# Weaving the units of two expert layers within a step, and a down projection by points

## The reference

```python
h = mab(I, x);  x1 = mab(x, h)                       # attention, x: (2, 11456, 128)
logits = xn @ en.T / tau                             # first router
out[mask] = gate_w[mask, None] * (relu(x[mask] @ w1[e]) @ w2[e])   # F = 1024
logits = x @ w_gate + modality_bias[modality_id]     # second router, same expert form
```

## Time and profile before

| | |
|---|---|
| median of 3 runs | 1131.33 us (1130.93 to 1133.27) |
| the profiled execution | 1135.07 us |
| its span, first to last instruction | 1133.3 us |
| TensorE, VectorE, ScalarE, GpSimd busy | 88%, 67%, 61%, 18% of the span |
| a step of the loop | 19.25 us, 42 of them in the loop |

### The profile page before, as it was taken

How to read it: one execution, slowest core, us unless ns; L and a number is a source line. 1 busy time by engine, 2 the same in 40 slices (tenths; PEclk the granted TensorE clock), 3 DMA queues, 4 the chain that set the end, 5 groups by cost and what they waited for, 6 DMA issues and landing times.

```text
span 1133.3 us, 28294 instructions
## 1 busy us (share of the span) xinstructions
PE 1001.1 (88%) x6551; PEld 510.2 (45%) x6551; DVE 758.2 (67%) x2211; ACT 686.4 (61%) x1656; POOL 198.7 (18%) x438
## 2 busy tenths in 40 slices
PE   5266446589999999999999999999999999999886
PEld 4144312245445454555455554454554545554342
DVE  3144457566767777777777686767677777777563
ACT  3134346356666676666666666666666766666453
POOL 2691000211111111111111111111111111111000
PEclk9688769699999999999999999999999999999998
DMA  4976665000110101010000010001001010100000
GB/s 129 275 225 218 215 215 172 22 20 28 27 28 19 36 19 32 23 29 26 27 27 27 27 27 27 27 27 27 27 19 35 18 33 22 29 25 20 21 11 20
DMA packets 68615, 64.70 MB, mean 57 GB/s; under 512 B 9570, under 2 KB 60770, under 8 KB 68568
## 3 DMA queue, kind: packets, MB, share of 16 engines
q1 hardware_dynamic: 68568, 64.11, 19.0%
HBM read 40.55 MB, written 23.55 MB: 57 GB/s over the span
## 4 chain that ended last, share of the span: by engine, by line
PE 81%; SPq 6%; DMA 5%; issue 3%; DVE 2%; ACT 2%; POOL 1%; ACTq 0%; DVEq 0%; POOLq 0%
PE y L1224 42%; PE up L1247 22%; PE up L1237 7%; DMA stage<-in_moe_w 2%; SPq L301 2%; DMA GW<-in_x 2%; PE y L1311 2%; SPq L303 2%; PE up L1163 1%; PE TB L1271 1%; PE SM L1295 1%; SPq L316 1%; PE SM L1283 1%; SPq L310 1%; PE TB L1259 1%
## 5 line engine op out<-in xcount | busy, mean ns | idle before, releaser
L811 DVE SCALAR_TENSOR_TENSOR hlo<-up,hhi 128x500 f16<-128x500 f32 x736 | 490.2, 672 | 205.5 <-ACT hhi L560 203.0
L560 ACT ACTIVATE hhi<-up 128x500 f16<-128x500 f32 x736 | 415.5, 586 | 143.3 <-PE up L1237 75.9
L1247 PE MATMUL up<-ytb,W1B 128*128 (+1 forms) x1104 | 277.7, 382 | 17.4 <-issue 14.8
L1224 PE MATMUL y<-hhi,W2A 128*128 128x500 f16 x736 | 217.1, 376 | 1.1 <-DVE hlo L811 1.1
L1224 PE MATMUL y<-hhi,GW 128*128 128x500 f16 x736 | 216.0, 374 | 0.5 <-DVE hlo L811 0.4
L1247 PEld LDWEIGHTS up<-ytb,W1B 128*128 x1104 | 108.6, 99 | 155.8 <-issue 48.2
L1237 PE MATMUL up<-E4T,GW 128*128 (+1 forms) x368 | 138.4, 380 | 0.0
L1224 PE MATMUL y<-hlo,W2A 128*128 128x500 f16 x368 | 137.8, 374 | 0.0
L1224 PE MATMUL y<-hlo,GW 128*128 128x500 f16 x368 | 137.6, 374 | 0.0
L476 POOL TENSOR_TENSOR st<-ss,root 125x4 f32<-125x4 f32 x46 | 46.8, 1018 | 374.5 <-ACT TB L592 374.5
L1224 PEld LDWEIGHTS y<-hhi,W2A 128*128 x736 | 67.8, 97 | 66.6 <-issue 15.5
(11 more groups left out here) (158 smaller groups left out, 1053.5 us busy)
## 6 DMA issues: line engine op xcount, KB each, us to landing
x_turned<-GW SPq DMA_DIRECT2D x46, 250.0 KB, 4.1
xth<-x_turned SPq DMA_DIRECT2D x46, 250.0 KB, 2.6
out<-yout SPq DMA_DIRECT2D x46, 250.0 KB
GW<-in_x SPq DMA_DIRECT2D x46, 240.0 KB
stage<-in_moe_w SPq DMA_DIRECT2D x16, 512.0 KB, 4.2
W1B<-in_moe_w SPq DMA_DIRECT2D x8, 512.0 KB, 7.2
w2s<-in_moe_w SPq DMA_DIRECT2D x8, 512.0 KB, 3.9
GW<-in_x SPq DMA_DIRECT2D x46, 10.0 KB
```

The costliest lines, as they stand in the source:

```text
L560: nc.scalar.activation(hhi[:, (u % UP) * CT:(u % UP + 1) * CT], ups[u % UP][:, 0:CT], ACT.Relu).then_inc(s["hi_done"], 1)
L811: nc.vector.scalar_tensor_tensor(hlo[:, o:o + CT], ups[u % UP][:, 0:CT], 0.0, hhi[:, o:o + CT], ALU.max, ALU.subtract).then_inc(s["lo_done ...
L1224: ins = mm(y[:, 0:CT], W[:, bass.ds(woff + (fb * 2 * C + o), C)], h[:, k * CT:(k + 1) * CT], start=opens and fb == 0 and n == 0, stop=fb = ...
L1247: ins = mm(ups[k][:, 0:CT], W1B[:, bass.ds(woff + (wl * F + fb * P), P)], ytb[:, bass.ds(yoff + yl * CW, CT)], start=n == 0, stop=n == 2)
```

## The change

1. The order of TensorE's units in a step with both layers becomes 0, 1, 8, 2, 3, 9, 4, 5, 10, 6, 7, 11, 12, 13, 14, 15: layer one's first three units stand between layer two's. Buffers and tasks go by position, no longer by unit.
2. Layer two's down takes the hidden activations as the stationary operand and the weights as the moving one: 12 matmuls of 128 columns with a weight load each, in place of 3 of 500. Its output has points on partitions, so `yT`, its copy and the four transposes go.
3. ScalarE's squares are split over positions 4 and 5; the result's four parts stand at 13 (two), 14 and 15; exps moves from 13 to 11. The factor 1/S_OUT moves into `coef` on VectorE.
4. The second router moves to position 1. `hhi` and `hlo` get 4 columns of padding a slot, cleared once by GpSimd ahead of the pipeline.

```diff
+        hhi, hlo = (sb(n, [P, UP * CW], f16)[:, :] for n in ("hhi", "hlo"))
-        yT = sb("yT", [P, CT])[:, :]
+        WOVEN = (0, 1, 8, 2, 3, 9, 4, 5, 10, 6, 7, 11, 12, 13, 14, 15)
...
-            for m in (ytb, E4T):
+            for m in (ytb, E4T, hhi, hlo):
                 nc.gpsimd.memset(m[:, :], 0.0).then_inc(s["pads_cleared"], 1)
... (ScalarE)
-                def squares():
+                def squares(h):
                     act.wait_ge(s["att_done"], p + 1)
-                    for j in range(TJ):
+                    for j in range(h * TJ // 2, (h + 1) * TJ // 2):
...
-                def yt(after):
-                    act.wait_ge(s["pass_done"], after)
-                    nc.scalar.activation(yT[:, :], y2[:, 0:CT], ACT.Copy, scale=1.0 / S_OUT).then_inc(
...
+                def result(j, after):
+                    if j == 0:
+                        act.wait_ge(s["gate_steps"], CG * (c + 3))
+                        act.wait_ge(s["out_free"], c + 1)
+                        act.wait_ge(s["pass_done"], after)
+                    ins = nc.scalar.activation(yout[:, j * C:(j + 1) * C], y2[0:TQ, j * C:(j + 1) * C], ACT.Copy,
+                                               scale=coef[:, bass.ds(parity(c) * TJ + j, 1)])
...
-                            8: [lexps] if rx or ry else [], 10: [lambda: yt(after())] if l2 else [],
-                            13: [exps] if xq else [], 15: [result] if l2 else []}
+                            5: [lambda: squares(1)] if rx else [], 8: [lexps] if rx or ry else [],
+                            11: [exps] if xq else [], 13: part(0) + part(1), 14: part(2), 15: part(3)}
... (TensorE)
+                def down_by_point(woff, opens):
+                    def down(fb, k):
+                        if fb == 0 and opens:
+                            pe.wait_ge(s["result_ready"], c + 1)
+                        for n, (h, o) in enumerate(((hhi, C), (hhi, 0), (hlo, 0))):
+                            for j in range(TJ):
+                                ins = mm(y2[:, j * C:(j + 1) * C], h[:, k * CW + j * TQ:k * CW + j * TQ + P],
+                                         W2B[:, bass.ds(woff + (fb * 2 * C + o), C)],
...
-                def out_transposes():
...
-                tasks = {1: when(rx, first_router), 2: when(ry, second_router),
-                         7: when(xq, scores), 8: when(joint, counts), 12: when(l2, out_transposes)}
+                tasks = {1: when(rx, first_router) + when(ry, second_router),
+                         7: when(xq, scores), 8: when(joint, counts)}
...
+                        if n == 2:
+                            us = [us[k] for k in WOVEN]
```

More of the change, by code:

```diff
@@ L608, in exps, with part @@
                         s["chunk_exp"], 1)
[L610 to L617, removed]
-                def tasks(after):
-                    return {1: [e4t] if rx else [], 4: [squares] if rx else [],
-                            8: [lexps] if rx or ry else [], 10: [lambda: yt(after())] if l2 else [],
-                            13: [exps] if xq else [], 15: [result] if l2 else []}
+                def result(j, after):
[5 more added lines that the diff above has]
+                                               scale=coef[:, bass.ds(parity(c) * TJ + j, 1)])
+                    if j == TJ - 1:
+                        ins.then_inc(s["result_ready"], 1)
+                def tasks(after):
+                    def part(j):
+                        return [lambda: result(j, after())] if l2 else []
+                    return {1: [e4t] if rx else [], 4: [lambda: squares(0)] if rx else [],
+                            5: [lambda: squares(1)] if rx else [], 8: [lexps] if rx or ry else [],
+                            11: [exps] if xq else [], 13: part(0) + part(1), 14: part(2), 15: part(3)}
                 def step(mixed):
@@ L956, in factors @@
                         hold(v, "result_ready", c + 1)
-                        tell(nc.vector.tensor_tensor(coef[:, now], gs[:, 1, 1, :], c1[:, now], ALU.mult), "gate_steps")
+                        tell(nc.vector.scalar_tensor_tensor(coef[:, now], gs[:, 1, 1, :], 1.0 / S_OUT, c1[:, now], ALU.mult,
+                                                            ALU.mult), "gate_steps")
                     else:
@@ L1179, in units @@
             def units(base, us, tasks, start=()):
-                for u, up, _down, _last in us[:UP]:
-                    up(u % NF, u % UP).then_inc(s["up_done"], 1)
+                first = us[0][0]
+                for k, (u, up, _down, _last) in enumerate(us[:UP]):
+                    up(u % NF, k).then_inc(s["up_done"], 1)
                 for task in start:
@@ L1192, in units @@
                         w, up = us[k + UP][:2]
-                        up(w % NF, w % UP).then_inc(s["up_done"], 1)
-                    for task in tasks.get(u, ()):
+                        up(w % NF, k % UP).then_inc(s["up_done"], 1)
+                    for task in tasks.get(first + k, ()):
                         task()
@@ L1249, in up @@
                         return ins
-                    def before():
-                        pe.wait_ge(s["result_ready"], c + 1)
-                    return up, down_of(W2B, woff, y2, opens, before if opens else None)
+                    return up, down_by_point(woff, opens)
                 def e4():
```

33 lines of the change are left out of this document (15 added, 18 removed).

## The result

| kernel | median us | runs | ratio to before (95% interval) |
|---|---|---|---|
| before | 1131.32 | 1130.93 to 1133.27 | |
| changed | 1191.05 | 1189.42 to 1194.47 | 1.052 (1.049 to 1.0551) |

A forecast was written before the change was run, and what follows sets the result against it. TensorE was taken as the bound, with a new wait for the last `hlo` at each step's end: 44 steps x 0.60 = 26.4, less 1.7 at the edges, +24.7, so 1131.3 becomes 1156 us, range 1118 to 1182.

The forecast's parts named there:

- The routers at position 1 find `e4t` done: Middle of the step: `e4t` is ready at t = 3.35, the routers need it at 4.55; no cost entered.
- A down by points 0.68: Layer two's downs on TensorE: 0.68 us each, +0.05 apiece, +0.40 a step (from +0.1 to +2.9).
- The rival with 0.0825 a pair: Weight loads don't hide in long runs: 0.99 a down, 2.5 a step more, 1265 us; chance 0.09.
- Idle time ahead of position 14: End of the step: result parts delay relu 14 and 15, so TensorE idles 0.84 us for the last `hlo`.
- The rival in which the parts don't hold relu up: End of the step: ScalarE does the result's parts under TensorE's work; +0.15 a step, 1136 us; chance 0.12.
- The next step's start: Step's end: next first up 1.69 us after the last `hlo`, at 19.86, so each step is 0.60 longer.
- The stalls at 7 and 8 gone: Middle of the step: the weave removes TensorE's two waits for `hlo`, 0.26 us.
- Transposes gone, -0.44: End of the step: dropping the `yT` transposes saves 0.44 us of TensorE and 0.59 of ScalarE.
- The norm's edge at 0: Middle of the step: VectorE waits about 0.4 in `norm`, `hlo` of position 6 just in time; cost 0 (up to +0.15).
- The code at 0: TensorE's loop body grows by some 400 instructions; cost 0, bound a stall of 2.45 us in every step.
- the rival of a stall in each iteration: The loop no longer fits the instruction buffer: 42 x 2.5 = +105, 1260 us; chance 0.03.
- The other side, 1116: TensorE stays the bound, stalls gone, last `hlo` before t = 17.3: -0.30 a step, 1116 us; faster had chance 0.15.

The follow-up runs named there:

- E7: Changed kernel with the second router reading one fixed half of its input, so no address computed at run time: 1158.15 us, ratio 1.0231.
- E1: Changed kernel with the second router back at position 2: 1168.65 us, ratio 1.031.
- E3: Changed kernel with the old order of units 0 to 15, all else of the change kept: 1151.04 us, ratio 1.0162.
- E2: Changed kernel with all four result parts at position 15, behind relu 15: 1176.29 us, ratio 1.0379.
- E8: Kernel before with the downs of positions 14 and 15 each waiting for their own `hlo`: 1121.11 us, ratio 0.99.
- E6: Kernel before with one edit, the second router at position 1: 1136.11 us, ratio 1.0043.
- E5: Changed kernel with the old order of units, second router at position 2 and all result parts at 15: 1148.69 us, ratio 1.0149.
- E11: Kernel before with own `hlo` waits for the downs of positions 14 and 15, and the second router at position 0, ahead of the first: 1127.1 us, ratio 0.9946.
- E10: Changed kernel with second router at position 2, result parts at 15, and own `hlo` waits for the downs of 14 and 15: 1130.84 us, ratio 0.9977.

## Why the prediction was wrong

It had 1156 with a range of 1118 to 1182; the kernel takes 1191. The direction was right and the size less than half: the forecast was 24.7, the medians differ by 59.7 and the spans by 54.3.

**The step that failed** is "The routers at position 1 find `e4t` done": with that the moved router was given no cost at all. It asked of the moved router only whether its data was there in time, and the data was. It didn't ask when TensorE's sequencer would get there. The second router has more address computations at run time than any other part of the step, eight, and these were free only because the sequencer ran about a microsecond ahead of the array. In the changed kernel the sequencer waits for `hlo` of position 1 (VectorE ends it at 629.58 + 0.67 = 630.25), and then has the addresses of the down, of one up and of the first router to compute before it comes to the second's at 631.7. This wait ends as it did before the change, 3.31 after the step's first up; but the weave has taken 0.84 of ups from ahead of the router, so the array is there at 631.86, with most of the second router's computations (631.7 to 632.7) still to come. Shown by E7 (0.81 gone with the computations), by E1 (0.63 gone with the place), by E3 (0.52 gone with the order) and by the changed kernel's own written-out step with constant addresses (0.30). All but the first of the loop's 42 steps pay 0.80 on average; the first pays 0.07, and the written-out ones, with constant addresses, nothing. That is 33 us; 1156 + 33 = 1189, and E7, the changed kernel without it, ran in 1158. The row that should have raised the question was there: the router's line has run-time slices, and the trace of before lists its computations over 0.9 us against 0.31 of matmuls. I had counted the router by its matmuls.

The other steps, one by one:

- **A down by points 0.68** (0.67 measured; 0.31 a step, 0.35 with the E4 transposes ahead of the first, against 0.40). The rows of four pairs carried over to rows of twelve: twelve in 0.67 is 0.056 us each. The rival with 0.0825 a pair falls.

  The Trainium skill's figure ("TensorE: Matmul & The Clock Gate", section "Back-to-back issue gap"), some 81 ns for a weight load and a 128-column matmul in a stream, isn't what this kernel does: the row 634.25 to 634.92 is below it, and the measurement decides.
- **Idle time ahead of position 14**: 0.84 forecast, 0.74 measured, with the releaser named, and relu 14 behind two parts of the result. The mechanism holds, by E2, whose 0.34 is the parts' share; the remainder is the bare chain up, relu, `hlo`. The rival in which the parts don't hold relu up falls.
- **The next step's start**, 1.69 behind the last `hlo`: 625.27 + 1.69 = 626.96, measured 626.94. Before, the same distance rules, which E8 shows: with the wait divided, the step shortens by 0.23.
- **The stalls at 7 and 8 gone**: right in size (-0.26), and the cause holds as far as it goes: E7, woven and with nothing lost at the router, has no stall there (TensorE waits for `hlo` once a step, ahead of position 14). But the weave isn't needed for it. E3 and E6 lose them with the order of before, where TensorE loses about 0.3 us at the router; E5 and E11, with that order and nothing lost, keep them. So what the forecast counted as a gain of the weave was to be had without it, and in the changed kernel the router's 0.81 alone would have done.
- **Transposes gone, -0.44**: entered as work saved. E5 shows that the saving is given back at once as idle time for `hlo`. In the forecast it vanished inside the chain that I followed at the end of the step, so no number was wrong by it; but the change had nothing to win there.
- **The norm's edge at 0**: VectorE waits 0.32 there, TensorE not at all; in the changed kernel it comes 0.8 late by the router, but in E10, only 0.2 late, it doesn't wait either. **The code at 0**: between 350 and 1050 us the changed kernel has no instruction DMA, and the queue has 28 packets in all, above; the rival of a stall in each iteration falls. The steps written out behind the loop do pay more: ahead of their first ups, five waits released by "issue" add up to 17.0 us, against 11.8 before. No run shows what of that is the longer code.
- **The other side, 1116**: its two stalls went, and its condition, the last `hlo` before t = 17.3, failed as forecast: it ends at 18.83, and at 17.97 in E7, without the router's loss.

The sum of what was foreseen: 0.60 forecast, less 0.05 for the downs (with the E4 transposes), 0.10 for the idle time and 0.02 at the start of the step, is 0.43 a step; with the 0.81, 1.24, which is what the step grew by. Over the kernel the forecast of 24.7 gets 33 from the router and loses 7 by the rest of the step; the 3.6 left to the spans' 54.3 lie at the edges, on top of the -1.7 that I had for them. The lower clock there and the waits above are what the traces show; how much is whose stays open. E1 and E10 show that such edges differ by 5 to 7 us from one build to the next.

## What to carry to other kernels

An instruction's place has two dues: when its data is there, and when the issuing sequencer gets to it with what it has to compute on the way. Before moving a group with run-time addresses, look up its register operations in the trace and what wait lies ahead of them: a sequencer that has just been released has no lead to hide them under. Work taken out of a stretch that ends in another engine's chain buys nothing, and a wait that asks for later results than its own instruction needs holds back all that is issued behind it; dividing one here was worth 0.23 us a step, and the whole change with its losses mended (E10) doesn't come up to that.

## What the hardware showed that I had not expected

- A run-time address costs TensorE's sequencer far more than its record says: the records are 46 ns long and start 0.13 us apart, and leaving eight of them out gave back 0.81 us (E7). The same weight loads and matmuls with fixed addresses follow one another every 0.026 us. And a down of 24 instructions put the computations behind it no later than one of six did (E3, E6): address computations were what the sequencer's time went into there, not plain instructions.
- Exposed sequencer time looks like busy TensorE. The twelve 8-column matmuls are "1.08 busy" with no idle time ahead, because overlapping records of 0.166 to 0.178 us fill the gaps. Only the distance between starts, 1.12 against 0.31, tells.
- Slowing TensorE in one place repaired a stall in another: E6 added 0.36 us at the router and lost 0.29 of stalls, a net of 0.07 us a step.
